# Retention with two MLPs: combined weights stored and reloaded, block sums in PSUM, sums of x from PSUM, another order in the prologue and in the first quad

## The reference, cut to what matters

```python
q, k, v: (4, 8, 768, 64)                       # batch, heads, time, head width
for t in range(768):                           # retention, one decay per head
    state = gamma * state + outer(k[t], v[t])
    y[t] = q[t] @ state / 8
x = y as (3072, 512)                           # 4 * 768 rows, 8 * 64 columns
x = (h * cos(h)) @ w1_out, h = x @ w1_in       # layer 1: (512, 2048), (2048, 512)
out = G(h) @ w2_out,       h = x @ w2_in       # layer 2
# G(h) = h for h >= 1, 0 for h <= -1, (h + 1)^2 / 4 between
```

## Time and profile before

| | |
|---|---|
| timed runs, median | 1201.3 us |
| profiled execution | 1205.87 us, its span 1204.1 us |
| mean granted TensorE clock | 0.974 |
| busy: TensorE, VectorE, ScalarE, GpSimd | 1126.1, 785.4, 560.8, 601.2 us |
| busy: TensorE weight loads (beside the matmuls) | 900.2 us |
| DMA | 78.88 MB, mean 66 GB/s |

### The profile page before, as it was taken

The page is one execution under the profiler, slowest core; times in us unless marked ns, Lnnn a source line. Parts: engine busy times, 40 slices in busy tenths (PEclk is TensorE's granted clock), DMA queues, the critical chain, the costliest instruction groups (busy, mean ns, idle before and its releaser), DMA issues.

```text
span 1204.1 us, 14743 instructions
## 1 busy us (share of the span) xinstructions
PE 1126.1 (94%) x5572; PEld 900.2 (75%) x5572; DVE 785.4 (65%) x1002; ACT 560.8 (47%) x892; POOL 601.2 (50%) x585
## 2 busy tenths in 40 slices
PE   6779888998999989899998899999999999999998
PEld 5657766776777767777776678888788887888887
DVE  5577777446677754567774878665676676677642
ACT  2245756423666742366664444444444434444332
POOL 3567567136466513645650767552465545355400
PEclk8779999999999999999999899999999999999999
DMA  9012121241100134220014121113011112111000
GB/s 354 7 36 70 35 70 60 81 159 52 71 28 26 36 108 155 71 71 24 30 36 150 60 105 36 35 36 122 13 58 35 35 52 89 53 35 36 18 36 35
DMA packets 42726, 78.88 MB, mean 66 GB/s; under 512 B 4512, under 2 KB 4640, under 8 KB 42656
## 3 DMA queue, kind: packets, MB, share of 16 engines
q1 hardware_dynamic: 42656, 77.95, 18.9%
HBM read 65.35 MB, written 12.58 MB: 65 GB/s over the span
## 4 chain that ended last, share of the span: by engine, by line
PE 51%; DVE 23%; ACT 17%; issue 6%; DMA 2%; POOL 1%; SPq 0%; ACTq 0%; DVEq 0%
PE bank L435 7%; PE bank L437 7%; PE bank L436 7%; DVE g_lo L575 7%; PE bank L402 6%; PE bank L406 6%; PE bank L404 6%; ACT work L769 5%; DVE work L545 4%; ACT work L771 4%; ACT tw L725 4%; DVE x_lo L534 3%; PE bank L431 2%; PE bank L354 2%; PE bank L432 2%
## 5 line engine op out<-in xcount | busy, mean ns | idle before, releaser
L402 PE MATMUL bank<-x_hi,tw 128*128 128x512 f32 x672 | 272.0, 405 | 21.2 <-ACT work L744 11.5
L924 POOL TENSOR_TENSOR tw<-raw,tw 128x896 fp32r<-128x896 f32 x96 | 204.7, 2141 | 165.6 <-ACT tw L725 165.6
L404 PE MATMUL bank<-x_lo,tw 128*128 128x512 f32 x672 | 268.3, 399 | 0.0
L406 PE MATMUL bank<-x_hi,tw 128*128 128x512 f32 x672 | 268.2, 399 | 0.0
L431 PE MATMUL bank<-g_hi,wd_hi 128*128 128x512 f32 x384 | 159.0, 414 | 28.5 <-DVE g_lo L575 24.2
L575 DVE SCALAR_TENSOR_TENSOR g_lo<-late,g_hi 128x512 fp32r<-128x512 f32 x96 | 87.6, 913 | 147.8 <-ACT g_hi L785 147.8
L402 PEld LDWEIGHTS bank<-x_hi,tw 128*128 128x128 f32 x672 | 128.4, 191 | 62.5 <-ACT work L744 19.2
L575 DVE SCALAR_TENSOR_TENSOR g_lo<-work,g_hi 128x512 fp32r<-128x512 f32 x96 | 130.5, 1360 | 41.2 <-ACT g_hi L785 38.4
L432 PE MATMUL bank<-g_lo,wd_hi 128*128 128x512 f32 x384 | 153.2, 399 | 0.0
L433 PE MATMUL bank<-g_hi,wd_lo 128*128 128x512 f32 x384 | 153.1, 399 | 0.0
L406 PEld LDWEIGHTS bank<-x_hi,tw 128*128 128x128 f32 x672 | 128.5, 191 | 30.6
(11 more groups left out here) (81 smaller groups left out, 1770.0 us busy)
## 6 DMA issues: line engine op xcount, KB each, us to landing
raw<-in_w1u SPq DMA_DIRECT2D x48, 256.0 KB, 2.8
raw<-in_w2u SPq DMA_DIRECT2D x48, 256.0 KB, 2.8
work<-x_scratch SPq DMA_DIRECT2D x24, 256.0 KB, 3.1
wd_raw<-in_w1d SPq DMA_DIRECT2D x8, 512.0 KB, 4.7
q_sb<-in_q_t SPq DMA_DIRECT2D x16, 256.0 KB, 3.7
k_sb<-in_k_t SPq DMA_DIRECT2D x16, 256.0 KB, 3.8
kn_sb<-in_k_n SPq DMA_DIRECT2D x16, 256.0 KB, 2.6
v_sb<-in_v_n SPq DMA_DIRECT2D x16, 256.0 KB, 3.1
```

The lines of the kernel that those rows point to most:

```text
L402: nc.tensor.matmul(to[:, :], w[:, kt, 0, i, :], x_hi[:, i, kt, :], start=opens, stop=False, skip_group_check=True)
L404: nc.tensor.matmul(to[:, :], w[:, kt, 0, i, :], x_lo[:, i, kt, :], start=False, stop=False, skip_group_check=True)
L406: last = nc.tensor.matmul(to[:, :], w[:, kt, 1, i, :], x_hi[:, i, kt, :], start=False, stop=kt == 1, skip_group_check=True)
L924: nc.gpsimd.tensor_tensor(tw[half][:, kt, 1, :, :], raw[half][:, kt, 1, :, :], tw[half][:, kt, 0, :, :].bitcast(F32), ALU.subtract).then_i ...
```

## The change

**Weights.** Combined weights, high and low, are made only in spans 0 and 3 (the first of each layer) and each quad's are stored to DRAM (`t_scratch`, `store_t`). In the other four spans `load_weights` loads them straight into `tw`, 2 x 7 KB per partition and kt, and GpSimd's `t_sums` and `t_low` and ScalarE's `t_high` are not issued. It waits for p3 of quad n - 2 and, behind a made quad, for its store.

**Block sums in PSUM.** A fourth bank is in use; `sum_h22`, `sum_h21`, `sum_h12` write into PSUM banks (except H22 of quad 0 and H21, H12 of quad 7, which stay in `work`), and `turns`, `angle` and `gate` read them there. So p1, p6 and p5 wait for gates 0, 1 and 2 of the quad before (p6 of quad 1 only for `sum_u2`).

**Sums of x.** `split_high` and `split_low` read the attention's output from PSUM where no sum is needed; the sums (`x_sum`) are VectorE's, with one operand in PSUM. Only six of eight outputs are copied. In layer 2 the sums stay on GpSimd.

**Order.** In the prologue and beside the tails scores(u + 2) or scores(u + 1) and the next mask come before the outer product and the state update; q of units 2 to 7 is scaled on GpSimd, which also clears the state. p1 and p7 of quad 0 are issued before unit 7. Quad 0 of every span runs p1, p7, p6, p2, p5, p4, p3. k and v are loaded apart, v into two buffers. Layer 2's first two down weight loads are issued before the row stores and the x loads. The diff, cut to its core:

```diff
         def quad_banks(s, q):
-            return [up_banks(s)[(3 * q + i) % 4] for i in range(3)]
+            order = ((0, 3, 2, 1), (0, 3, 1, 2), (0, 2, 3, 1), (0, 1, 2, 3))[q if q < 1 else (q - 1) % 3 + 1]
+            return [up_banks(s)[i] for i in order]
+
+        def hidden(s, q, k):
+            bank_1, bank_2, bank_3, bank_4 = quad_banks(s, q)
+            if q == 0:
+                return (bank_1[:, :], work[:, H22, :], bank_4[:, :], bank_3[:, :])[k]
+            if q == QUADS - 1:
+                return (bank_1[:, :], bank_4[:, :], work[:, H21, :], work[:, H12, :])[k]
+            return (bank_1[:, :], bank_4[:, :], bank_2[:, :], bank_3[:, :])[k]
+
+        def made(s):
+            return s % PAIRS == 0
+
...
+            def load_weights(n):
+                span, q, i = n // QUADS, n % QUADS, n % 2
+                layer = span // PAIRS
                 if n >= 2:
                     sp.wait_ge(product_done["p3"], n - 1)
-                if n % QUADS == 1 and n // QUADS in (1, 2):
-                    sp.wait_ge(y_done, AHEAD * (n // QUADS + 1))
-                    sp.wait_ge(outer_done, min(AHEAD * (n // QUADS + 1), UNITS - KT))
+                    if made((n - 2) // QUADS):
+                        sp.wait_ge(t_stored[i], 16 * (place_made(n - 2) + 1))
+                if q == 1 and span in (1, 2):
+                    sp.wait_ge(y_done, AHEAD * (span + 1))
+                    sp.wait_ge(outer_done, min(AHEAD * (span + 1), UNITS - KT))
                 for kt in range(2):
-                    sp.dma_start(raw[n % 2][:, kt, 1, 0:4, :], up_input[layer][q, kt]).then_inc(raw_in[n % 2][kt], 16)
+                    if made(span):
+                        sp.dma_start(raw[i][:, kt, 1, 0:4, :], up_input[layer][q, kt]).then_inc(raw_in[i][kt], 16)
+                    else:
+                        sp.dma_start(tw[i][:, kt, :, :, :].bitcast(F32), t_scratch[layer][q][:, kt, :, :, :]).then_inc(t_in[i][kt], 16)
+
+            def store_t(n):
+                layer, q, i = n // (QUADS * PAIRS), n % QUADS, n % 2
+                sp.wait_ge(tlo_done, weight_item(n, 1) + 1)
+                sp.dma_start(t_scratch[layer][q], tw[i][:, :, :, :, :].bitcast(F32)).then_inc(t_stored[i], 16)
 
...
                 elif s + 1 < SPANS:
                     load_x2(s + 1, 0)
+                if s == PAIRS - 1:
+                    load_wd(1, 0)
                 store_rows(s, 1)
...
+                    if s == PAIRS - 1:
+                        load_wd(1, 1)
                     load_x2(s + 1, 1)
                 if s == PAIRS - 1:
-                    for q in range(QUADS):
+                    for q in range(2, QUADS):
...
                 if q == 0:
                     pe.wait_ge(xlo_done, NS * s + max(m for m in range(NS) if SPLITS[m][0] == name) + 1)
-                if name == "p1" and q >= 2:
-                    pe.wait_ge(h12_done, n - 1)
-                if name == "p6" and q >= 1:
+                    if name in ("p7", "p4"):
+                        to = bank_4
+                    if name == "p6" and s < PAIRS:
+                        pe.wait_ge(state_done, 2 * min(AHEAD * (s + 1) - (s == 0), UNITS - KT))
+                    if name == "p5" and s < PAIRS:
+                        y_taken(AHEAD * (s + 1) - 1 - (s == 0))
+                elif name == "p1":
                     pe.wait_ge(g_done, 4 * (n - 1) + 1)
-                if name == "p5" and q >= 1:
-                    pe.wait_ge(h21_done, n)
+                elif name == "p6":
+                    if q == 1:
+                        pe.wait_ge(u2_done, n)
+                    else:
+                        pe.wait_ge(g_done, 4 * (n - 1) + 2)
+                elif name == "p7":
+                    pe.wait_ge(u2_done, n + 1)
+                elif name == "p5":
+                    pe.wait_ge(g_done, 4 * (n - 1) + 3)
                 if name == "p2":
                     pe.wait_ge(p1_copied, n + 1)
...
             for u in range(AHEAD):
                 outputs(u)
-                outer(u)
                 if u + 2 < AHEAD:
                     scores(u + 2)
+                outer(u)
+                if u == AHEAD - 2:
+                    pe.wait_ge(masked, 2 * (AHEAD - 1))
+                    for name in EARLY_PRODUCTS:
+                        product(0, 0, name)
             for s in range(SPANS):
                 if s == 0:
...
                     pe.wait_ge(rows1_done, 4 * s)
                 for q in range(QUADS):
+                    if q == 0:
+                        for name in FIRST_PRODUCTS if s else LATER_PRODUCTS:
+                            product(s, q, name)
+                        continue
                     product(s, q, "p1")
...
                     down(s, *tail.pop(0))
                     for i in range(AHEAD):
                         outputs(u + i)
+                        if i + 1 < AHEAD:
+                            scores(u + i + 1)
                         outer(u + i)
                         if i + 1 < AHEAD:
-                            scores(u + i + 1)
                             for _ in range(BETWEEN[i]):
                                 down(s, *tail.pop(0))
...
+            def x_sum(s, which, kt):
+                u = AHEAD * s + (4 if which == "s3" else 6) + kt
+                to, other, op = {"s3": (X11, X11, ALU.subtract), "s2": (SUM2, X11, ALU.subtract), "s1": (X21, X21, ALU.add),
+                                 "s4": (X12, X12, ALU.subtract)}[which]
+                to, other = work[:, to + kt, :], work[:, other + kt, :]
...
+                    dve.wait_ge(x_copied, COPIES * s + KT + kt + 1)
+                y = unit_banks(u)[2][:, :]
+                nc.vector.scalar_tensor_tensor(out=to, in0=y, scalar=SCALE, in1=other, op0=ALU.mult, op1=op,
+                                               reverse1=which == "s3").then_inc(summed, 1)
...
+            def operands(s, i, lows=()):
+                kt, lows = i % 2, list(lows)
+                if i in (4, 5):
+                    x_sum(s, "s3", kt)
+                if i < 6:
+                    split_low(s, i)
+                    return
+                x_sum(s, "s2", kt)
+                x_sum(s, "s1", kt)
+                split_low(s, SPLITS_OF[i][0])
+                split_low(s, SPLITS_OF[i][1])
+                if lows:
+                    gate_low(s - 1, *lows.pop(0))
+                split_low(s, SPLITS_OF[i][2])
+                x_sum(s, "s4", kt)
+                if lows:
+                    gate_low(s - 1, *lows.pop(0))
...
             def sum_h21(s, q):
                 n = QUADS * s + q
                 dve.wait_ge(product_done["p4"], n + 1)
-                nc.vector.tensor_tensor(work[:, H21, :], quad_banks(s, q)[1][:, :], work[:, S1, :],
-                                        ALU.add).then_inc(h21_done, 1)
+                if q == QUADS - 1 and s:
+                    dve.wait_ge(rows1_out[2], 16 * s)
+                bank, other = (quad_banks(s, q)[3], U2) if q == 0 else (quad_banks(s, q)[1], S1)
+                nc.vector.tensor_tensor(hidden(s, q, 2), bank[:, :], work[:, other, :], ALU.add).then_inc(h21_done, 1)
 
...
+                    sum_u3(s, q)
+                    gate(s, q, 0)
                 sum_h22(s, q)
+                if q == 0:
+                    gate(s, q, 0)
                 gate_low(s, 1, q)
                 angle(s, q, 1)
                 gate(s, q, 1)
...
+            mask(0)
             scale_q(1)
-            for p in range(1, KT):
-                nc.vector.memset(state[:, p, :, :], 0.0).then_inc(zeroed, 1)
             dve.wait_ge(zeroed, KT)
             for u in range(AHEAD):
-                mask(u)
-                if u + 2 < AHEAD:
-                    scale_q(u + 2)
+                if u + 1 < AHEAD:
+                    mask(u + 1)
                 update_state(u)
-                if 1 <= u <= 4:
...
 
+            nc.gpsimd.memset(state[:, 0, :, :], 0.0).then_inc(zeroed, 1)
             nc.gpsimd.memset(half_one[:, :], 0.5).then_inc(halves, 1)
+            for p in range(1, KT):
+                nc.gpsimd.memset(state[:, p, :, :], 0.0).then_inc(zeroed, 1)
             pool.wait_ge(table_first, 16)
             pool.wait_ge(table_in, 16)
-            for u in range(5):
+            for u in range(AHEAD):
+                if u >= 2:
+                    scale_q(u)
                 scale_k(u)
-            t_sums(0)
-            t_sums(1)
-            scale_k(5)
-            t_low(0)
-            scale_k(6)
-            t_low(1)
...
+                    t_sums(0)
+                    t_sums(1)
+                if u in (6, 7):
+                    t_low(u - 6)
             for s in range(SPANS):
                 for q in range(QUADS):
-                    i = 2 * (QUADS * s + q + 1)
```

357 lines of the change are left out of this document (200 added, 157 removed).

## The result

The kernel after took 1146.31 us, median of four runs (1145.91 to 1149.71); the kernel before, run on the same chip beside it, 1203.97 us (four runs, 1200.32 to 1206.66). The ratio is 0.9529, with a 95% interval of 0.9492 to 0.9567: 57.7 us less, where 63.6 were forecast. The profiled execution took 1146.63 us, its span 1144.8, against 1205.87 and 1204.1 before.

The account below looks back on a forecast made before the run. TensorE bounds the kernel wherever work is at hand; its idle time comes from GpSimd contention with VectorE and the ScalarE/VectorE chain. Terms sum to -63.6 from the median 1201.3: 1137.7, given as 1137, range 1122 to 1170.

Parts of the forecast that it names:

- the reload was not late: Denies the late-reload rival: a quad's pair of weight loads takes 19.5 us, 4.3 too long, in 28 quads, 1257 us; chance 0.04.
- the rival that the prologue stays put: Prologue: GpSimd's contended scalings, sums and t_lows take nearly as long as the old chain; only 5 of 17 us come, 1149; 0.14.
- Start, -17 forecast: Start until quad 1's p2: new unit order and q scalings on GpSimd take it from 86.2 to 69 us.
- Span 0's quads, -13.4: Span 0's other quads: H22's angle loses 2.2 us, 16.1 us a quad, 122.0 to 108.6 us in all.
- Gates in PSUM, 1.6 us of margin: Spans 1 and 2: p6 must wait for gate 1, which was to end 1.6 us before p6.
- the two terms of 0.94 and 1.5 us: Spans 1 and 2, ahead of gate 1: weight copies of 0.94 us and the low half's GpSimd stretch of 1.5 both go.
- The rival of the chain: Layer 1: gate 1 late for p6 by 1 us in 18 quads, half the tails' stops stay; about 1160, 1164 at worst; 0.14.
- Tails 0 and 1, -8.5 and -9.9: Tails 0 and 1, 93.0 and 89.4 us: both fall to TensorE's busy time, 84.5 and 79.4.
- Spans 1 and 2, -5 each: Quads of spans 1 and 2: 121.7 us each falls to 117, 504 matmuls at layer 2's rate.
- Tail 2, -4.8: Tail 2, 65.4 us: ScalarE's 4.51 us wait for wd_raw goes, its load issued ahead of row stores and x loads.
- Layer 2, 0: Layer 2, 504.6 us: TensorE-bound, dearer clamp hidden; rival that VectorE's PSUM reads set it, 12.6 us, 1150, chance 0.04.
- The reload, 5 to 8 us to land, no cost: A quad's weights, 2 x 917.5 KB, land in 5 to 8 us, hidden within one quad's 15.2 us.

Follow-up runs that it names:

- the second one: Another profile of the kernel before, unchanged but for an empty line: 1198.23 us in one run, start to quad 1's p2 77.2 us.
- the table of four: Spans 1 and 2's quads, weights made in each span or reloaded: 243.4 or 233.4 us with the rest as before, 245.7 or 234.3 as after.
- the one execution of 3838.62 us: One execution of the kernel after with a second DRAM-to-DRAM copy of all reloaded weights; its other executions took 1144.35 to 1146.31 us.
- the doubled reload: The kernel after with a second DRAM-to-DRAM copy of each quad's stored weights ahead of each reload: 1145.49 us, ratio 0.9514.

## Why the prediction was right, and where it was off

The time lay 9 us over the forecast and within its range, and no rival came: the reload was not late, GpSimd was relieved, the chain held p6 in no quad for over 0.5 us, and layer 2 stood. The start is the closest case: it moved by 14.9 us against the profile read, but by only 5.9 against the second one, near the 5 of the rival that the prologue stays put. p1 at 43.0 us, short of that rival's 48, and the run with the old order of the unit speak against it. The margin is also helped by the profile that was read: against the second one, the profiled spans differ by 51.7 us, not 59.3. By its steps:

**Start, -17 forecast; -14.9 against the profile read.** Two errors meet here. The term's base was one execution with the granted clock at 0.71 in its middle: 86.2 us where a second profile gives 77.2. Against that one the change gains 5.9, not 14.9. The text took 69 "for a slow clock (0.80 here)"; the clock after was 0.88, so the allowance covered the result but not the base. The order of the unit is what does the most: undone, the stage is 85.3 us. The second error: GpSimd's list was added up as if it were always at work, with "2 us of waits for data and ScalarE". One wait for ScalarE alone was 5.74 us, and behind it stood unit 7's q, which TensorE then waited for. The text had p1 at 38 to 41; it was at 43.0, and 38.6 with that q moved ahead. p6 came at 53.9 (49 forecast); p2, which stands ahead of it in this quad, had waited 2.03 us for ScalarE's copy of p1, a wait in no term.

**Span 0's quads, -13.4; measured -15.8.** The mechanism as told: the angle lost its 2.2 us, 16.02 us a quad (16.1 forecast), 18.13 with the sums in SBUF. That the average fits so well is partly luck, since it mixes one period of 17.64 with five of 15.7. The last quad gave 3.0 us where 1.1 was forecast: before, TensorE waited 2.7 us at its end for the last piece of the down weights from GpSimd, and after it does not. The rest over 15.3 was put down to VectorE's low half beside GpSimd, rightly: once t_low starts behind the low half, that takes 0.69 us in place of 1.33 and the period is 15.25.

**Gates in PSUM, 1.6 us of margin in spans 1 and 2.** Gate 1 ends 2.1 us before p6 there in span 1's quads 3 to 7, 0.4 before quad 2's. In span 0 TensorE's wait for it is at most 0.4 us, six times (`DVE late L705`). Without the reload the margin is gone, 12 waits and 5.2 us in spans 1 and 2, as the two terms of 0.94 and 1.5 us had said. The rival of the chain (p6 late in 18 quads) did not come.

**Tails 0 and 1, -8.5 and -9.9; measured -6.2 and -7.6.** This is the step that failed. The text took both tails at TensorE's busy time and looked for new cost in unit 6's operands, 1 to 3 us. That was small: 0.21 us before one outer product and 1.1 before one group of the down products. It left out the queue that supplies the scores. A step was moved ahead on TensorE, while q's scaling still stood behind k's on GpSimd, and k's load behind the outer product. Moving q ahead gave 4.4 and 2.2 us back, and with it both tails are 82.4 and 79.6, at or under the figures forecast.

**Spans 1 and 2, -5 each; measured -4.6 and -4.5.** Right, and the table of four shows that the reload alone does it. The sum was generous: 114.3 us at layer 2's rate is 117.7, not 117, so its own working gave -4.0.

**Tail 2, -4.8; measured -5.5.** Right, by the cause named; undone, the stage is 4.3 us longer than after.

**Layer 2, 0; measured -0.1.** The clamp from PSUM took 683 ns for 515 and hid under TensorE. The Trainium skill (VectorE: DVE Perf Modes, section "Rules for kernel authors") leaves the choice between the slower mode on a PSUM source and a copy to SBUF first, the latter when many operations follow. By that rule alone, as the prediction priced it, layer 2 would have lost 12.6 us; its stage shows no loss. In span 0, beside a working GpSimd, sums kept in SBUF made the quads 14.5 us longer.

**The reload, 5 to 8 us to land, no cost.** 6.3 us, and none at 11.0.

**The 9 us in all.** 2.7 are the level: the median of before was 1201.3 in the runs shown and 1203.97 beside the kernel after. 0.7 are the rounding to 1137. The rest is the gain, 57.7 for 63.6 by the medians and 59.3 by the profiled spans. Those 4.3 us are, to rounding, the tails' 4.6, the start's 2.1 and 0.9 in the quads of spans 1 and 2, less 2.4 in span 0 and 0.8 in tail 2 and layer 2.

What stays open: why the clock fell in one profile of the prologue before and not in the other; the 17 us from quad 1 to quad 2 of span 0; and the one execution of 3838.62 us. No run took back the sums of x on VectorE, the scores ahead of the outer product in the tails, or the order of quad 0 in the later spans, so what each of them gave is not shown.

## What to carry to other kernels

When a step moves ahead on the engine that sets the time, write down what it consumes and move that on each queue that supplies it, loads and scalings alike: an in-order engine gives the new order only as far back as its slowest neighbour in line. Two remedies for the same contention aren't added: find which stretch each one serves, since here the reload paid only where GpSimd had gone silent and the PSUM operands only where it had not. And before a stage's length serves as a base, look at a second profile of the same kernel, above all where the granted clock of the stage is under 1.

## What the runs showed of the hardware

VectorE reading one operand in PSUM and writing its result there took 0.70 us for 128 x 512, against 0.69 with the result in SBUF, and a GpSimd memset of that size 0.52 us; both had been in no row of before:

```profile
L751 DVE TENSOR_TENSOR bank<-bank,work 128x512 f32<-128x512 f32 x42 | 29.2, 696 | 14.3 <-PE bank L493 14.3
...
L1102 POOL MEMSET state<- 128x512 f32 x3 | 1.4, 524 | 0.0
```

Of the angles that still read SBUF alone (H22 of quad 0, H21 and H12 of quad 7), only the first, H22 in span 0, met GpSimd's subtraction, as in the earlier trace rows: it took 2.86 us from 63.85 us on and ended 0.5 us after the subtraction, which took 2.83 from 63.35 on. The other eight took 0.68 to 0.69 us.

And DMA traffic of 119 GB/s in span 1's quads, or 229 with the doubled reload, left the pace of TensorE where it was: 117.1 and 117.2 us for that stage.
